# Gram products as 64x64 results, and two accumulations split into two passes by row pairs, in the recurrence of an attention and expert kernel

## The reference, cut to what matters

```python
for t in range(S):                                    # S = 768; per batch (4) and head (8)
    y[:, :, t] = einsum('bhd,bhde->bhe', r_t, state)  # state is 40 x 40
    Sa = einsum('bhde,bhe->bhd', state, a_t)
    state = state * w_t[:, :, None, :] - einsum('bhd,bhe->bhde', Sa, b_t)
    state = state + einsum('bhd,bhe->bhde', v_t, k_t)
```

## Time and profile before

| | us |
|---|---|
| median of three runs | 1461.15 |
| the runs | 1460.15, 1464.88, 1461.15 |
| the profiled execution, its own time | 1462.92 |
| its span on the core | 1461.1 |

### The profile page before, as it was taken

The page is one execution under the profiler, slowest core; times in us unless marked ns, Lnnn a source line. Parts: engine busy times, 40 slices in busy tenths (PEclk is TensorE's granted clock), DMA queues, the critical chain, the costliest instruction groups (busy, mean ns, idle before and its releaser), DMA issues. The chain is left out here.

```text
span 1461.1 us, 37835 instructions
## 1 busy us (share of the span) xinstructions
PE 1270.4 (87%) x15278; PEld 1159.1 (79%) x15278; DVE 947.4 (65%) x1619; ACT 666.1 (46%) x1453; POOL 304.3 (21%) x262
## 2 busy tenths in 40 slices
PE   4458789778887966999999999999939999999998
PEld 3447577666776755999999999999938888888987
DVE  8978685795938017788788788887825535455343
ACT  3325444444543330567666676776603333333332
POOL 1116262542623221111111111111042012020000
PEclk9998888888988875999999999999969999999999
DMA  6563535536243312877877778778521011010000
GB/s 228 143 161 99 144 119 139 169 111 167 92 113 114 91 25 71 259 239 226 263 229 248 254 210 265 246 226 254 167 77 42 23 33 54 1 54 18 0 19 18
DMA packets 158832, 197.61 MB, mean 135 GB/s; under 512 B 62869, under 2 KB 117373, under 8 KB 158717
## 3 DMA queue, kind: packets, MB, share of 16 engines
q1 hardware_dynamic: 136724, 148.12, 33.5%
q10 hardware_dynamic: 16713, 29.77, 6.5%
q0 software_dynamic: 5280, 18.03, 4.3%
HBM read 171.57 MB, written 24.31 MB: 134 GB/s over the span
## 5 line engine op out<-in xcount | busy, mean ns | idle before, releaser
L350 DVE TENSOR_TENSOR prod<-Tl,Lt 128x1 f32<-128x1 f32 (+30 forms) x186 | 151.9, 817 | 51.4 <-DMA Lt<-lscr 45.3
L1297 DVE TENSOR_TENSOR gf<-psM,low 128x512 f32<-128x512 f32 x96 | 66.3, 691 | 181.1 <-ACT low L1335 169.4
L1335 ACT ACTIVATE low<-psM 128x512 f32<-128x512 f32 x96 | 57.5, 599 | 244.3 <-PE psM L1393 223.5
L1001 PE MATMUL psE<-w2h,hh 128*128 128x320 f32 x496 | 155.7, 314 | 0.0
L1003 PE MATMUL psE<-w2h,hl 128*128 128x320 f32 x496 | 153.3, 309 | 0.0
L1002 PE MATMUL psE<-w2l,hh 128*128 128x320 f32 x496 | 153.2, 309 | 0.0
L1089 POOL DMA_INDIRECT xs<-xrow,src x62 | 60.9, 982 | 410.2 <-PE psE L970 370.8
L986 PE MATMUL psE<-xh,w1h 128*128 128x256 f32 x496 | 141.1, 285 | 1.9 <-DVE xh L833 1.9
L987 PE MATMUL psE<-xl,w1h 128*128 128x256 f32 x496 | 141.0, 284 | 0.0
L988 PE MATMUL psE<-xh,w1l 128*128 128x256 f32 x496 | 140.9, 284 | 0.0
L833 DVE TENSOR_TENSOR w2l<-w2t,w2h 128x320 fp32r<-128x320 f32 x248 | 122.0, 492 | 16.3 <-ACT w2h L828 16.3
(11 more groups left out here) (185 smaller groups left out, 3154.8 us busy)
## 6 DMA issues: line engine op xcount, KB each, us to landing
w2t<-in_w_dram SPq DMA_DIRECT2D x31, 1280.0 KB, 6.8
w1t<-in_w_dram SPq DMA_DIRECT2D x31, 1024.0 KB, 8.9
w1t<-in_w_dram SPq DMA_DIRECT2D x62, 256.0 KB, 9.4
Vd<-in_vG_dram ACTq DMA_DIRECT2D x44, 320.0 KB, 4.8
ysort<-ys SPq DMA_DIRECT2D x31, 320.0 KB, 5.0
RV<-in_rvE_dram ACTq DMA_DIRECT2D x44, 208.0 KB
P<-in_wR_dram SPq DMA_DIRECT2D x24, 209.6 KB
U<-in_wE_dram SPq DMA_DIRECT2D x24, 209.6 KB
```

The costliest lines, as they stand in the source:

```text
L350: mark(nc.vector.tensor_tensor(prod[:, 0:t, 0:t], Tl[:, 0:t, CH - t:CH], Lt[:, t:t + 1, CH - t:CH].to_broadcast([128, t, t]), ALU.mult))
L1001: mm(o, hh[:, f, sl], w2h[:, f, :], start=(f == 0), stop=False)
```

## The change

The grams (`lb`, `lk`) and `gp`: each 128x128 product becomes two 64x64 products, the two diagonal quarters that hold all used blocks. A group has 16 matmuls with 64 columns in place of 8 with 128, and each goes to one of four quarters of the array (`E_[p]` picks the rows, `T_[j]` the columns). `grow_K` and `add_B` split the contraction over 128 partitions into two of 64, whose other columns are zero anyway: 16 matmuls of 80 (64) columns in place of 8 of 160 (128). They run in two passes of 8, so that in one pass no two row halves write the same bank. The second pass of `grow_K` comes behind `solve` and waits for the first (`o_S`), and in the first chunk of a slice the first pass waits for the copy of the state into banks 0 and 1 (`o_in`). The second pass of `add_B` comes behind `grow_B`, just ahead of `add_K`.

```diff
@@ -568,6 +568,7 @@
             turn = nc.tensor.transpose
             E_ = [slice(64 * h, 64 * h + D) for h in range(2)]
             Z_ = [slice(CH * h, CH * h + CH) for h in range(4)]
+            T_ = [slice(64 * j, 64 * j + 64) for j in range(2)]
             unit = ident[0:EP, 0:EP]
 
             def first(k):
@@ -605,8 +606,10 @@
                 pe.wait_ge(q["e_B"], 2 * s + c // 2 + 1)
                 for b in range(NB):
                     for p in range(2):
-                        m = mm(ps[:, bank + p, 128 * b:128 * b + 128], flat(AT[E_[p], s % 3, c, 4 * b:4 * b + 4, :]),
-                               BT[E_[p], s % 2, 3 - c, 4 * b:4 * b + 4, :], start=True, stop=True)
+                        for j in range(2):
+                            o, g = 128 * b + 64 * j, 4 * b + 2 * j
+                            m = mm(ps[T_[j], bank + p, o:o + 64], flat(AT[E_[p], s % 3, c, g:g + 2, :]),
+                                   BT[E_[p], s % 2, 3 - c, g:g + 2, :], start=True, stop=True)
                 m.then_inc(q["p_G"], 1)
 
             def lk(s, c):
@@ -615,8 +618,10 @@
                 pe.wait_ge(q["e_K"], s + 1)
                 for h in range(4):
                     for p in range(2):
-                        m = mm(ps[:, bank + p, 128 * h:128 * h + 128], flat(KT[E_[p], s % 2, 3 - c, 4 * h:4 * h + 4, :]),
-                               AT[E_[p], s % 3, c, h:16:4, :], start=True, stop=True)
+                        for j in range(2):
+                            o, g = 128 * h + 64 * j, 4 * h + 2 * j
+                            m = mm(ps[T_[j], bank + p, o:o + 64], flat(KT[E_[p], s % 2, 3 - c, g:g + 2, :]),
+                                   AT[E_[p], s % 3, c, h + 8 * j:h + 8 * j + 5:4, :], start=True, stop=True)
                 m.then_inc(q["p_G"], 1)
 
             def tok(s, c):
@@ -665,13 +670,16 @@
                                    RV[E_[x], k % 3, 0, 8 * i + 4 * p + h, :], start=(f == 0 and h == 0), stop=False, skip_group_check=True)
                 m.then_inc(q["o_y"], 1)
 
-            def grow_K(k):
+            def grow_K(k, f):
                 s, c = slot(k)
-                for h in range(4):
+                for u in range(2):
                     for p in range(2):
-                        o = (h % 2) * NB * D
-                        m = mm(ps[E_[p], h // 2, o:o + NB * D], Kk[:, (4 * s + c) % RT, h, p, :], Vd[:, k % 2, p, h, :],
-                               start=False, stop=True, skip_group_check=True)
+                        for i in range(2):
+                            h = 2 * (i ^ f) + u
+                            o = u * NB * D + 2 * D * i
+                            m = mm(ps[E_[p], i ^ f, o:o + 2 * D], Kk[T_[i], (4 * s + c) % RT, h, p, :],
+                                   Vd[T_[i], k % 2, p, h, 2 * D * i:2 * D * i + 2 * D],
+                                   start=False, stop=True, skip_group_check=True)
                 m.then_inc(q["o_S"], 1)
 
             def grow_B(k):
@@ -685,14 +693,17 @@
                                    start=False, stop=True, skip_group_check=True)
                 m.then_inc(q["p_S"], 1)
 
-            def add_B(k):
+            def add_B(k, f):
                 s, c = slot(k)
-                for b in range(NB):
+                for u in range(2):
                     for p in range(2):
-                        o = (b % 2) * 128
-                        m = mm(ps[E_[p], 2 + b // 2, o:o + 128], Bk[:, (4 * s + c) % RT, b, p, :], Gpb[:, b, p, :],
-                               start=False, stop=True, skip_group_check=True)
-                m.then_inc(q["o_y"], 1)
+                        for j in range(2):
+                            b = 2 * (1 - (j ^ f)) + u
+                            o = 128 * u + 64 * j
+                            m = mm(ps[E_[p], 2 + b // 2, o:o + 64], Bk[T_[j], (4 * s + c) % RT, b, p, :], Gpb[T_[j], b, p, T_[j]],
+                                   start=False, stop=True, skip_group_check=True)
+                if f == 0:
+                    m.then_inc(q["o_y"], 1)
 
             def add_K(k):
                 s, c = slot(k)
@@ -708,8 +719,10 @@
             def gp(k):
                 for i in range(4):
                     for x in range(2):
-                        m = mm(ps[:, 6 + x, 128 * i:128 * i + 128], PTs[E_[x], i, :],
-                               RV[E_[x], k % 3, 0, 4 * i:4 * i + 4, :].rearrange("p g t -> p (g t)"), start=True, stop=True)
+                        for j in range(2):
+                            o, g = 128 * i + 64 * j, 4 * i + 2 * j
+                            m = mm(ps[T_[j], 6 + x, o:o + 64], PTs[E_[x], i, T_[j]],
+                                   RV[E_[x], k % 3, 0, g:g + 2, :].rearrange("p g t -> p (g t)"), start=True, stop=True)
                 m.then_inc(q["p_Gp"], 1)
 
             pe.wait_ge(q["z_v"], 2)
@@ -759,12 +772,16 @@
                     turn_S(k)
                     if c == 0:
                         for i in range(2):
-                            mm(ps[0:EP, i, 0:320], unit, S0T[:, 2 * i:2 * i + 2, :, 0:D].rearrange("p h b d -> p (h b) d"),
-                               start=True, stop=False, skip_group_check=True)
-                    grow_K(k)
+                            m = mm(ps[0:EP, i, 0:320], unit, S0T[:, 2 * i:2 * i + 2, :, 0:D].rearrange("p h b d -> p (h b) d"),
+                                   start=True, stop=False, skip_group_check=True)
+                        m.then_inc(q["o_in"], 1)
+                        pe.wait_ge(q["o_in"], s + 1)
+                    grow_K(k, 0)
                     pe.wait_ge(q["a_X"], k + 1)
                     pe.wait_ge(q["a_G"], before(k) + (1 if grams(k) else 0))
                     solve(k)
+                    pe.wait_ge(q["o_S"], 2 * k + 1)
+                    grow_K(k, 1)
                     pe.wait_ge(q["a_gv"], k + 1)
                     gram_of(1)
                 if k:
@@ -780,7 +797,7 @@
                     turn_P()
                 if k:
                     pe.wait_ge(q["g_gp"], k)
-                    add_B(k - 1)
+                    add_B(k - 1, 0)
                 if k < NK:
                     if s + 1 < NS_ and TOKS[c]:
                         pe.wait_ge(q["a_G"], before(k + 1))
@@ -791,11 +808,12 @@
                         rows(s - 1, 0)
                         rows(s - 1, 1)
                     pe.wait_ge(q["a_Pn"], k + 1)
-                    pe.wait_ge(q["o_S"], k + 1)
+                    pe.wait_ge(q["o_S"], 2 * k + 2)
                     grow_B(k)
                 if k:
                     pe.wait_ge(q["g_gv"], k)
                     pe.wait_ge(q["o_y"], 3 * k)
+                    add_B(k - 1, 1)
                     add_K(k - 1)
                 if k == NK:
                     break
```

More of the change, by code:

```diff
@@ L92, in stage_a @@
                  "z_v z_g e_A e_B e_K v_P v_U v_end v_dve v_inv v_y v_S "
-                 "o_S o_y p_X p_Gv p_G p_Str p_P p_tok p_rows p_PT p_S p_y p_Gp "
+                 "o_in o_S o_y p_X p_Gv p_G p_Str p_P p_tok p_rows p_PT p_S p_y p_Gp "
                  "a_X a_gv a_G a_S0 a_Pn a_tok a_row a_PT a_S a_Gp g_go g_lg g_lh g_lk g_gv g_gp").split()
```

## The result

The change makes the kernel slower. The median of six runs is 1476.36 us (1471.88 to 1481.49) against 1464.39 us for six runs of the kernel before (1460.15 to 1467.07): the ratio is 1.010, with a 95% interval of 1.0078 to 1.0122. A second measurement of the changed kernel, beside its own runs of the kernel before, gave 1.0121, 1.0102 to 1.0141. The forecast was 1446 us, range 1437 to 1455: 15 us of gain were forecast and 12 us of loss came. The profiled execution took 1481.49 us; its span grew from 1461.1 to 1479.7 us.

The account below looks back on a forecast made before the run. Slices 0 to 3 bound by VectorE's inverse and its transfers, slice 5 by TensorE. Slice gains 3.4, 4.3, 4.3, 3.65, plus 1.0 (`Lt`), less 1.0 (late instructions): 15.6 us off 1462.92, less 1.8 (median): 1446 us, range 1437 to 1455.

Parts of the forecast that it names:

- the prices: Start to next start at full clock: grams and `gp` 0.60 us, `grow_K` 0.59, `add_B` 0.57.
- A: Rival, 12%: grams and `gp` don't get shorter, as weight loads wait for each other; gain 9.2 us, 1452 us.
- B: Rival, 4%: a floor per small matmul (estimated 25 ns) holds all four groups near 0.80 us; 1449.5 us.
- the first four stops of VectorE for TensorE: VectorE's waits for `y_out` in slices 0 to 3: to go or fall below 1 us.
- The fifth: VectorE's 8.48 us stop for `y_out` in slice 4: to fall by 4.3 us, to near 4.
- against it: 1.0 us: Cost put on TensorE's late instructions, from 96 to 160 more instructions per chunk: 1.0 us in all.
- Rival C: Rival, 10%: shorter work between the same waits lowers the clock to 0.85 in slices 4 and 5; 4.8 us, 1450.5 us.
- the twelve grams there are worth nothing: Ahead of the loop TensorE waits 23.9 us for `KT` from VectorE, so shorter grams there gain nothing.
- slices 0 to 3, forecast 7.7 us shorter: Shorter stops of VectorE for `y_out`: slice 0 gains 3.4 us, slices 1 to 3 together 4.3.
- The last part of the forecast: VectorE's wait for `Lt`: earlier TensorE parts the next chunks' loads from these transfers, 0 to 3.5 us gain, 1.0 taken.
- E: Rival, 6%: late-instruction stops of 1.7 us, once or twice more in each of eleven chunks, add 28 us: 1473 us.
- D: Rival, 12%: one more late-instruction stop of 1 us in half to two thirds of eleven chunks; 1451 to 1453 us.

Follow-up runs that it names:

- before_pad: Kernel before, plus 24 one-column matmuls ahead of `lkv` in each chunk, with hardly any work; 1479.34 us, ratio 1.0117.
- new_in_slices_0_3: Changed forms in chunks 0 to 15 only, old forms elsewhere, against the kernel before; 1459.84 us, ratio 1.0009.
- all_but_first_twelve: Changed kernel with the twelve grams ahead of the loop in the old form, against the kernel before; 1465.88 us, ratio 1.0038.
- only_add_B: Kernel before with `add_B` alone in two passes, against the kernel before; ratio 0.9977.

## Why the prediction was wrong, point by point

**Right: what bounds the kernel, and the prices.** Grams were forecast at 0.60 and take 0.47 to 0.62 us; `add_B` in two passes, at 0.57, takes 0.36 and 0.23 (440.06 to 440.42 and 443.50 to 443.73 in the trace). `grow_K` takes 0.72 where 0.59 was forecast, `gp` 0.56 and 0.57 (429.88 to 430.44, 528.89 to 529.46) for 0.60. The account of work confirms the sum: for slices 4 and 5 the prices give 8 x 1.45 + 4 x 0.49 = 13.6 us of TensorE work less, and 12.5 and 14.1 were measured. Rivals A and B, that the groups don't shorten, fall. The floor of 25 ns that B names is there all the same, elsewhere: the one-column matmuls of before_pad, which all go to one place of the array, start 25 ns apart, record by record, while the 32 records of a group on four quarters start 15 to 23 ns apart.

**Right: the first four stops of VectorE for TensorE go.** They fell from 3.47, 2.51, 2.06 and 0.99 us to one of 1.23. The fifth, 8.48, which was to fall to near 4, stayed:

```profile
119.26 0.69 DVE L374 TENSOR_TENSOR xT<-psA,U 104x512 f32<-104x512 f32 x1 [1.23 <-PE psA L714]
...
446.42 0.69 DVE L374 TENSOR_TENSOR xT<-psA,U 104x512 f32<-104x512 f32 x1 [8.65 <-PE psA L638]
```

**Failed first: "against it: 1.0 us" for late instructions.** The prediction saw the stops of TensorE with no releaser, read them as late instructions, counted 96 to 160 more instructions for each chunk, and put 1.0 us on it. The term is 7 to 10 us in slices 4 and 5 alone (10.2 and 12.9 us for 3.3). The count was right and the price wasn't worked out. It could have been worked out from rows and packets of the kernel before: `read_S` runs 64 records with their 64 weight loads in 1.03 us, so a packet of 256 instructions is used up in some 2.1 us of such a stream. And a stop ends 2.3 to 3.1 us after the next packet starts to come in: this is so for all stops of 0.8 us and more in the two loops, 8 before the change and 25 after, where after the change a packet comes every 5.4 us on average. It bears out the reading as late instructions. A stream of small matmuls thus eats instructions about as fast as they arrive, and each group that was cut in two makes it denser. The longest stop shows it. The timeline of TensorE, and the DMA queues from 347 us and from 351.9 us on:

```profile
347.38 0.34 PE L579 MATMUL psA<-S0T,AT 40*32 40x40 f32 x23 [0.16 <-PE psA L599]
354.55 0.75 PE L579 MATMUL psA<-S0T,AT 40*32 40x40 f32 x41 [6.83 <-issue]
```
```profile
q1 hardware_dynamic: 566, 1.04, 67.5%
q10 hardware_dynamic: 123, 0.25, 19.1%
```
```profile
q10 hardware_dynamic: 193, 0.38, 47.2%
q1 hardware_dynamic: 180, 0.33, 39.9%
q8 instruction: 1, 0.02, 2.8%
```

TensorE stops at 347.72, in the midst of `first`. Until 351.9 no packet of instructions moves, while the DMA engines are 87% busy with `Vd`, `KT` and other loads; then one comes, and at 354.55 TensorE goes on. That the packet queued behind this traffic is likely, and was not tried. The Trainium skill, Runtime: NRT & Kernel Launch, Instruction fetch mechanics, says that an engine's instructions come in blocks of 256 (16 KiB) through a DMA queue of its own, and that this is hidden because the engine issues them more slowly than the blocks arrive. The 256 instructions and 16.4 KB agree with this trace; that it is hidden does not, with 64.1 us of such stops in the loop.

**Failed next: the clock was taken as it was.** Rival C went down to 0.85 in slices 4 and 5, priced at 4.8 us and given 10%. The clock came out at 0.84 and 0.78, and the time at 1.2 GHz rose from 22.6 to 42 to 48 us, a loss of 10 to 13. The prediction had argued that shorter work between the same waits may lower it. The runs show more: before_pad has more work than the kernel before and idles about as long (17.6 us of 143.2 for 16.9 of 125.3), and its clock fell all the same, although TensorE's waits for VectorE in these slices fell from 12.6 to 3.9 us. And the sum took the clock of slice 4 to come back at 414 us as before; that stretch at 1.2 GHz is 10.2 us long before and 20.5 us after the change (409.1 to 429.6), with TensorE busy 8.91 of the 9 us from 420 on and no late instruction in it (in the second measurement slice 4 has two such stretches of 10.2 us). The sum was thus made at prices at full clock, and 41.9 of TensorE's 105.6 busy us then ran at half clock.

**Failed as well: "the twelve grams there are worth nothing".** They lie ahead of TensorE's wait for `KT`, and the prediction looked at their time alone. In the old form of these twelve the changed kernel is 9 to 12 us faster, more than half of its loss. What they change is where the instructions behind them stand; the prediction has no term for it.

**Failed too: slices 0 to 3, forecast 7.7 us shorter, are 7.4 us longer** (319.2 to 326.6). VectorE's operations over these slices, kernel after (idle time ahead of them, and its releaser, last):

```profile
L350 DVE TENSOR_TENSOR prod<-Tl,Lt 128x1 f32<-128x1 f32 (+30 forms) x124 | 120.2, 970 | 41.1 <-DMA Lt<-lscr 37.2
L374 DVE TENSOR_TENSOR xT<-psA,U 104x512 f32<-104x512 f32 x14 | 9.5, 681 | 1.2 <-PE psA L714 1.2
...
L335 DVE RECIPROCAL start<-P 104x4 f32<-104x4 f32 x16 | 2.9, 180 | 14.5 <-DMA U<-in_wE_dram 14.1
```

Of the same rows before, L374 stood idle for 9.0 us ahead of it, L350 was busy 112.9 us, with 34.3 us of waits for `Lt`, and L335 waited 10.5 us for `U`. The stops for TensorE gave 7.8 us back, as the prediction said, and the circle took 7.3 (L350), 2.9 (`Lt`), 3.6 (`U`) and 1.8 us (the read of `tscr`, 9.8 for 8.0): 15.6 in all. The last part of the forecast, that `Lt` would come sooner, has the wrong sign. Why the transfers and the operations of the inverse got longer is not shown; new_in_slices_0_3, with nearly the same instructions in these slices, has them at 319.1, all_but_first_twelve, with the very same loop, at 315.9, and only_add_B at 320.6, so it may go with where the stops fall more than with the change itself; with some 5 us between executions of the same matmuls, more can't be said.

**The rivals.** E named the right side, the right resource and nearly the right time (1473), but with one mechanism where there are two of like size. It decides, it said, from 1.5 us more for each exposed chunk; the late instructions came to some 1 us for each (7 to 10 us over eight chunks), below that point, and the clock made up the rest. With 6% it was rated far too low, and C, D and E should have been weighed as one case: before_pad shows that added small matmuls bring both the lower clock and the late instructions. That its time came so near is luck: it had 28 us of late instructions in eleven chunks. The signs given for it ("stops with no releaser of 20 us and more", "a clock under 0.86") were the right ones.

**What stays open.** How much is clock and how much late instructions can't be parted further. Some of the time at the lower clock stands right behind a stop (1.4 us after the one that ended at 503.33 the clock fell for 10.2 us), some without one, as at the start of slice 4, and the fillers that were to hold the clock did not, or cost as much as they gave. That slices 0 to 3 are slow with one layout of the instructions and less so with others was seen, not explained.

## What to carry to other kernels

Cutting matmuls into quarters that run side by side saves array time and doubles the instructions; where a loop already runs streams of matmuls of some 16 ns each, look first at the stops with no releaser and at the granted clock, and price both, since here 12.5 us of saved work cost 19 us in these two. Try such a change in the stretch where TensorE is the path, by itself: 896 instructions there made it 10 us longer. And measure a second layout of the same code, moved by a hundred instructions or more, before you believe a difference under 1% in a kernel of this kind.

## What the runs showed of the hardware

- The same loop ran 0.4% or 1.2% slower than the kernel before, with 384 instructions fewer or more ahead of it.
- 24 matmuls of one column for each chunk, 1104 records and 30.7 us busy in the loop, lowered the granted clock of slices 4 and 5 from 0.89 and 0.88 to 0.85 and 0.84, and cost 18 us. TensorE was busy 125.6 of 143.2 us, and 39.8 us of that ran at 1.2 GHz.
- These one-column matmuls start 25 ns apart, record by record, at 2.4 GHz; the 64 records of `read_S`, on four quarters of the array, 16 ns apart.
- Instructions come to TensorE in packets of 256 (16.4 KB), and 33 of 33 stops of 0.8 us and more without a releaser, in the loops of the two kernels, ended 2.3 to 3.1 us after the start of a packet.
- Operations of VectorE on two inputs took several times as long beside one of GpSimd. The timelines of the two engines in the kernel after, VectorE first:

```profile
301.09 5.48 DVE L350 TENSOR_TENSOR prod<-Tl,Lt 128x441 f32<-128x441 f32 x1
...
309.67 0.71 DVE L350 TENSOR_TENSOR prod<-Tl,Lt 128x529 f32<-128x529 f32 x1
```
```profile
298.81 4.99 POOL L254 TENSOR_TENSOR KT<-KT,P 104x512 f32<-104x512 f32 x4
303.76 2.34 POOL L272 TENSOR_TENSOR Gpb<-Gpb,neg_m 128x1024 f32<-128x1024 f32 x1
306.06 1.09 POOL L265 TENSOR_TENSOR Gvb<-Gvb,two_m 128x256 f32<-128x256 f32 x1
```

441 elements took 5.48 us beside GpSimd, 529 took 0.71 us after it had ended. Later, 841 elements took 3.18 us beside an operation of GpSimd that began with it, and 784 just before took 0.98.
